# Block means of the values: GpSimd additions over a second load, in place of TensorE passes

## The reference, cut to what matters

```python
k_sum = k.reshape(B, H, nb, block, D).max(axis=3)
v_sum = v.reshape(B, H, nb, block, D).mean(axis=3)     # the block means of the values
scores_l = scale * np.matmul(q, k.transpose(0, 1, 3, 2))
scores_s = scale * np.einsum('bhsd,bhnd->bhsn', q, k_sum) + np.log(block)
...
a = softmax(concatenate([scores_l_masked, scores_s], axis=-1))
v_all = np.concatenate([v, v_sum], axis=2)
return np.matmul(a, v_all)
```

## Time and profile before

| | |
|---|---|
| median of 3 runs | 724.75 us (724.41 to 733.85) |
| the profiled execution: its own time | 723.32 us |
| its span | 721.5 us |
| PE busy | 625.3 us (87%) |
| DVE busy | 354.1 us (49%) |
| ACT busy | 259.9 us (36%) |
| POOL busy | 69.0 us (10%) |

### The profile page before, as it was taken

The page is one execution under the profiler, slowest core; times in us unless marked ns, Lnnn a source line. Parts: engine busy times, 40 slices in busy tenths (PEclk is TensorE's granted clock), DMA queues, the critical chain, the costliest instruction groups (busy, mean ns, idle before and its releaser), DMA issues.

```text
span 721.5 us, 11009 instructions
## 1 busy us (share of the span) xinstructions
PE 625.3 (87%) x3326; PEld 532.1 (74%) x3327; DVE 354.1 (49%) x890; ACT 259.9 (36%) x578; POOL 69.0 (10%) x96
## 2 busy tenths in 40 slices
PE   4899999710879899999849969999999999999994
PEld 3899999610658778878624448898899989988993
DVE  3577775572423452552235286644545454545442
ACT  2676775202313231441101114543344434443330
POOL 3121120015000010100100001002000040000001
PEclk9999999855889999999968988999999999999998
DMA  6444337017831481123150431000100010001001
GB/s 173 94 105 104 83 84 294 1 32 275 301 106 30 145 270 29 32 68 133 44 177 12 173 128 50 1 0 1 45 1 1 0 44 0 0 0 44 0 0 44
DMA packets 58297, 56.38 MB, mean 78 GB/s; under 512 B 43360, under 2 KB 43488, under 8 KB 57504
## 3 DMA queue, kind: packets, MB, share of 16 engines
q1 hardware_dynamic: 52480, 38.93, 17.7%
q0 software_dynamic: 3776, 13.44, 4.8%
q10 hardware_dynamic: 2016, 3.70, 2.3%
HBM read 41.04 MB, written 15.01 MB: 78 GB/s over the span
## 4 chain that ended last, share of the span: by engine, by line
PE 69%; DVE 8%; issue 8%; ACT 5%; DMA 4%; POOL 2%; SPq 2%; DVEq 1%; ACTq 0%; POOLq 0%
PE bank L1451 18%; PE bank L1438 17%; PE bank L1356 9%; PE bank L1328 6%; ACT arena L582 3%; DMA mid<-sorted_x 2%; PE bank L1381 2%; PE bank L1201 2%; DVE parts L935 2%; PE bank L1186 2%; POOL sorted_x L495 1%; PE bank L1210 1%; PE bank L1244 1%; PE bank L1394 1%; PE bank L1316 1%
## 5 line engine op out<-in xcount | busy, mean ns | idle before, releaser
L935 DVE TENSOR_TENSOR parts<-arena,parts 128x512 fp32r<-128x512 f32 (+1 forms) x152 | 111.3, 772 | 99.3 <-ACT parts L709 79.3
L1438 PE MATMUL bank<-parts 128*128 128x384 f32 x768 | 148.2, 342 | 2.1 <-DVE parts L935 2.0
L1451 PE MATMUL bank<-parts 128*128 128x512 f32 x576 | 143.7, 394 | 0.4 <-DVE mid L1095 0.3
L1438 PEld LDWEIGHTS bank<-parts 128*128 128x128 f32 x768 | 137.2, 190 | 8.1 <-DVE parts L935 4.0
L1451 PEld LDWEIGHTS bank<-parts 128*128 128x128 f32 x576 | 106.8, 188 | 21.0 <-DVE mid L1095 1.3
L1356 PE MATMUL bank<-parts 128*128 128x512 f32 x312 | 77.3, 405 | 6.2 <-DVE parts L935 5.3
L1328 PE MATMUL bank<-parts 128*128 128x512 f32 x312 | 76.1, 401 | 2.2 <-DVE parts L935 2.2
L1356 PEld LDWEIGHTS bank<-parts 128*128 128x128 f32 x312 | 59.6, 194 | 20.1 <-issue 4.8
L709 ACT ACTIVATE parts<-arena 128x512 fp32r<-128x512 f32 x64 | 40.4, 631 | 84.1 <-PE bank L1451 84.1
L1328 PEld LDWEIGHTS bank<-parts 128*128 128x128 f32 x312 | 59.0, 193 | 14.6 <-issue 2.8
L935 DVE TENSOR_TENSOR parts<-bank,parts 128x512 fp32r<-128x512 f32 (+1 forms) x56 | 35.2, 649 | 43.0 <-ACT parts L699 20.8
(11 more groups left out here) (171 smaller groups left out, 707.8 us busy)
## 6 DMA issues: line engine op xcount, KB each, us to landing
arena<-in_moe_w SPq DMA_DIRECT2D x24, 512.0 KB, 5.0
sorted_x<-mid POOLq DMA_DIRECT2D x1, 5160.0 KB, 17.5
arena<-in_moe_w_ch SPq DMA_DIRECT2D x2, 2048.0 KB, 8.3
arena<-in_moe_w_ch SPq DMA_DIRECT2D x4, 1024.0 KB, 9.0
mid<-sorted_x ACTq DMA_DIRECT2D x14, 258.0 KB, 3.2
arena<-in_k SPq DMA_DIRECT2D x16, 192.0 KB, 2.7
arena<-in_q SPq DMA_DIRECT2D x16, 192.0 KB, 3.2
x_all<-folded_y SPq DMA_DIRECT2D x6, 512.0 KB, 6.9
```

Source lines behind the costliest of these rows:

```text
L935: return dve.tensor_tensor(out, whole, upper.bitcast(F32), ALU.subtract)
L1438: last = pe.matmul(bank[2 + f % 2][:, 0:GN], w[:, f % 2, r], x[:, par, c, :], start=(c == 0 and w is m1_hi and x is cT_hi), stop=(c == DC ...
L1451: last = pe.matmul(bank[4 + t][:, :], x[:, f % 2, r], w[:, f % 2, :], start=(f == 0 and x is g_hi and w is m2_hi), stop=(f == MC - 1 and w ...
```

## The change

The averaging matrix, the 14 passes, their bank and their semaphore go. A second buffer `blocks` of two halves takes the values of a pair once more, in another layout: one block of 32 positions (32 x 64 numbers, 8 KB) to a partition, 24 partitions for each head, at the very partitions where the means belong in `vB`. GpSimd clears the buffer at the start. For each pair it adds the upper half of a partition's row to the lower half, four times over, and a fifth addition leaves 64 sums in `block_sum`. Each addition waits for the one before. ScalarE copies these sums into `vB` with the factor 1/32. For the first pair VectorE does the sum (a reduction over 32 x 64) and the two copies. The sums of pair i+1 stand on GpSimd right behind its columns of block maxima. The averaging matrix is 896 of the columns of the table of constants, which is now that much shorter.

```diff
@@ SyncE
+            def load_blocks(i, par):
+                for hh in range(2):
+                    lo = WB + (P - HB - NB) * hh
+                    vh = v_dram[bass.ds(2 * i + hh, 1)].rearrange("a (n j) d -> (a n) (j d)", j=BLOCK)
+                    sp.dma_start(blocks[lo:lo + NB, par, :], vh).then_inc(blocks_in[par], 16)
...
             sp.wait_ge(v_cleared, 2)
+            sp.wait_ge(blocks_set, 1)
+            load_blocks(0, 0)
             load_v(0, 0)
+            load_blocks(1, 1)
...
-            def next_pair(i, par):
+            def next_pair(i, par, more=True):
 
                 sp.wait_ge(qk_ps, 3 * (i + 1))
                 load_qk(i + 1)
                 sp.wait_ge(av_ps, ST * i + SIX)
                 load_v(i + 1, 1 - par)
+                if more:
+                    sp.wait_ge(vmean_ok, i + 1)
+                    load_blocks(i + 2, par)
@@ GpSimd
+            pool.memset(blocks, 0.0).then_inc(blocks_set, 1)
             pool.memset(vA, 0.0).then_inc(v_cleared, 1)
...
+            def block_sums(i, par):
+
+                pool.wait_ge(blocks_in[par], 32 * ((i + 2) // 2))
+                pool.wait_ge(vmean_ok, i)
+                pool.sem_inc(waited, 1)
+                n = BLOCK * D // 2
+                for step in range(4):
+                    pool.tensor_tensor(blocks[:, par, 0:n], blocks[:, par, 0:n], blocks[:, par, n:2 * n], ALU.add).then_inc(halved, 1)
+                    pool.wait_ge(halved, 4 * (i - 1) + step + 1)
+                    pool.sem_inc(waited, 1)
+                    n //= 2
+                pool.tensor_tensor(block_sum, blocks[:, par, 0:n], blocks[:, par, n:2 * n], ALU.add).then_inc(vsum_ok, 1)
+
             def keys_and_means(i, par):
                 windows(i, par)
                 block_max_columns(i, par)
+                block_sums(i, par)
@@ ScalarE
             def block_mean_rows(i, par):
 
-                act.wait_ge(vmean_ps, i + 1)
+                act.wait_ge(vsum_ok, i + 1)
                 for hh in range(2):
                     r = slice(WB + WB * hh, WB + WB * hh + WB)
-                    v_mean = Q_BANK[r, D * hh:D * hh + D].rearrange("p (a n) -> p a n", a=1).broadcast_to([WB, ST, D])
-                    last = act.activation(vB[r, par, :, hh, :], v_mean, ACT.Copy)
+                    v_sum = block_sum[r, :].rearrange("p (a n) -> p a n", a=1).broadcast_to([WB, ST, D])
+                    last = act.activation(vB[r, par, :, hh, :], v_sum, ACT.Copy, scale=1.0 / BLOCK)
                 last.then_inc(vmean_ok, 1)
...
-            block_mean_rows(0, 0)
@@ VectorE, ahead of the loop
+            dve.wait_ge(blocks_in[0], 32)
+            dve.tensor_reduce(block_sum, blocks[:, 0].rearrange("p (j d) -> p d j", d=D), axis=AX.X, op=ALU.add).then_inc(vsum_ok, 1)
+            dve.wait_ge(vsum_ok, 1)
+            dve.wait_ge(v_cleared, 2)
+            for hh in range(2):
+                r = slice(WB + WB * hh, WB + WB * hh + WB)
+                v_sum = block_sum[r, :].rearrange("p (a n) -> p a n", a=1).broadcast_to([WB, ST, D])
+                last = dve.tensor_scalar(vB[r, 0, :, hh, :], v_sum, 1.0 / BLOCK, None, ALU.mult)
+            last.then_inc(vmean_ok, 1)
@@ TensorE
-                    pe.wait_ge(v_in[par], 128 * ((i + 2) // 2))
-                    for t in range(ST):
-                        pe.matmul(Q_BANK[:, 0:P], block_mean[:, t, :], vA[:, par, t].rearrange("p h d -> p (h d)"), start=(t == 0), stop=False)
-                    pe.matmul(Q_BANK[:, 0:P], block_mean[:, ST, :], vB[:, par, ST - 1].rearrange("p h d -> p (h d)"),
-                              start=False, stop=True).then_inc(vmean_ps, 1)
...
                 if t == 0:
+                    pe.wait_ge(v_in[par], 128 * ((i + 2) // 2))
                     pe.wait_ge(vmean_ok, i + 1)
...
-                    if t in STAGE_AT and not last_pair:
-                        if t == 0:
-                            pe.wait_ge(vmean_ok, i + 1)
-                        stage(i + 1, 1 - par, STAGE_AT.index(t))
+                    if t < 3 and not last_pair:
+                        stage(i + 1, 1 - par, t)
```

More of the change, by code:

```diff
@@ L51 @@
 T_PRESENT, T_USED, T_COLS = T_EXP + E, T_EXP + E + 1, T_EXP + E + 2
-STAGE_AT = (0, 1, 2, 4)
 GATED = ((), (), (), (), (), (0,)), ((1,), (2,), (3,), (4,), (5, 6), (7, 8))
@@ L80, in shape_constants @@
     cols, at = {}, 0
-    for name, n in (("ident", P), ("mask", 3 * 2 * NS), ("block", 7 * 2 * HB), ("base", NT), ("forced", NT),
+    for name, n in (("ident", P), ("mask", 3 * 2 * NS), ("base", NT), ("forced", NT),
                     ("first", E), ("iota", 1), ("thr", NT), ("tri", E), ("slot", SLOTS + 1), ("ones", 1), ("odd", CW), ("expert", E), ("dest", NT), ("sum", P)):
@@ L100, in shape_constants @@
     put("mask", -np.stack([mask, second], 2))
[L102 to L111, removed]
     token = P * np.arange(NT)[None, :] + np.arange(P)[:, None]
@@ L181, in build @@
         mask = const("mask").rearrange("p (v h s) -> p v h s", v=3, h=2)
-        block_mean = const("block").rearrange("p (t n) -> p t n", t=7)
         class Cut:
@@ L211, in build @@
         xT_gate = mid[:, XW:XW + 1024].rearrange("p (b n) -> p b n", b=2)
+        blocks = mid[:, XW + 1024 + DM:XW + 1024 + DM + 2 * BLOCK * D].rearrange("p (b n) -> p b n", b=2)
         a = Cut(arena)
@@ L274, in build @@
         mean, var, rstd = (s(NT) for _ in range(3))
+        block_sum = s(D)
         fr = Cut(fou)
@@ L294, in build @@
         v_in = pair_of("v_in")
-        qk_ps, qk_sb, kmax_ok, ksum_ok, kwin_ok, vmean_ps, vmean_ok = sems("qk_ps qk_sb kmax_ok ksum_ok kwin_ok vmean_ps vmean_ok")
+        qk_ps, qk_sb, kmax_ok, ksum_ok, kwin_ok, halved, vsum_ok, vmean_ok = sems("qk_ps qk_sb kmax_ok ksum_ok kwin_ok halved vsum_ok vmean_ok")
+        blocks_set, = sems("blocks_set")
+        blocks_in = pair_of("blocks_in")
         s_ps, masked_ok, probs_ok, sum_ok, rinv_ok = sems("s_ps masked_ok probs_ok sum_ok rinv_ok")
@@ L381, in _ @@
                     next_pair(2 * step + par, par)
-            next_pair(PAIRS - 2, 0)
+            next_pair(PAIRS - 2, 0, False)
             w1_d = w1.rearrange("e (c p) n -> e p c n", p=P)
@@ L478, in keys_and_means @@
                 block_max_columns(i, par)
+                block_sums(i, par)
             pool.sem_inc(ksum_ok, 1)
-            keys_and_means(0, 0)
+            windows(0, 0)
+            block_max_columns(0, 0)
             with pool.Fori(0, PAIRS // 2 - 1) as step:
@@ L587, in attend @@
                         stage(i + 1, 1 - par, t - 1)
-                    if t == STAGE_AT[3] + 1 and not last_pair:
+                    if t == ST - 1 and not last_pair:
                         block_mean_rows(i + 1, 1 - par)
@@ L1180, in stage @@
                         last = turn(q_raw, 2 + t, P * t)
-                else:
-                    pe.wait_ge(qk_sb, 3 * i + 3)
-                    pe.wait_ge(consts_in, 16)
-                    pe.wait_ge(v_in[par], 128 * ((i + 2) // 2))
-                    for t in range(ST):
-                        pe.matmul(Q_BANK[:, 0:P], block_mean[:, t, :], vA[:, par, t].rearrange("p h d -> p (h d)"), start=(t == 0), stop=False)
-                    pe.matmul(Q_BANK[:, 0:P], block_mean[:, ST, :], vB[:, par, ST - 1].rearrange("p h d -> p (h d)"),
-                              start=False, stop=True).then_inc(vmean_ps, 1)
-                    return
                 last.then_inc(qk_ps, 1)
@@ L1225, in turn_gate @@
             def turn_gate(n):
-                if n == 0:
-                    pe.wait_ge(vmean_ok, PAIRS)
-                elif n <= EARLY:
+                if 1 <= n <= EARLY:
                     pe.wait_ge(lg_sb, n)
-                else:
+                elif n:
                     pe.wait_ge(xg_sb, n - 1)
@@ L1271, in _ @@
             scores(0, 0, 1)
-            stage(0, 0, 3)
             with pe.Fori(0, PAIRS // 2 - 1) as step:
```

## The result

The changed kernel takes 760.4 us (median of 4 runs, 759.35 to 764.23) against 724.6 us: 1.047 of the kernel before, 95% interval 1.038 to 1.056. The profiled execution has a span of 757.5 us against 721.5. That is slower, as forecast, but by 36 us and not by 21, and above the range.

What follows compares the result with a forecast made beforehand. TensorE was taken to bound the kernel, busy 87% of the span. 723.32 + 16.0 (waits) + 6.8 (clock) - 1.0 (start) = 745.1 us, forecast as 746 us since that execution is 1.43 us below the median; range 733 to 758.

Steps and rivals of the forecast that it cites:

- the order of the links: In each pair: GpSimd's additions behind its block-maxima columns, then ScalarE's rows of means and exponentials, then TensorE's turn; break-even 3.12 us.
- T: GpSimd, start of first addition to end of last: 2.9, 4.5 or 6.6 us by bounds, 5.4 taken.
- The hand-overs: Four waits between GpSimd's five additions, taken at half of 0.17 us each, 0.3 us for four.
- the wait: TensorE's turn of the next pair's first tile comes 2.28 us later; seven waits cost 16.0 us.
- The clock: TensorE idles 3.8 us before the turn; 1.7 us lost per clock fall, 4 of 7 taken, 6.8 us (0 to 11.9).
- The start: Before the loop, clearing, loads, pair 0's means and pair 1's keys: a gain of 1 us, ends -2 and +3.
- The loads in the loop: Two more DMAs of 192 KB in each pair, costed at nothing; without cover about 1 us in a pair.
- rival 1: The same wait before TensorE's turn without any fall of the clock: 739.8 us; chance 0.20.
- rival 2: Cheaper additions on GpSimd, 4.5 us, with one clock fall or none: 734 to 735 us; chance 0.16.
- rival 4: GpSimd's additions end before ScalarE wants them, TensorE's time is saved: 713 us, or 722; chance 0.07.
- rival 3: Dear additions on GpSimd, 6.6 us, and a clock fall in every pair: 760 us; chance 0.09.

Runs made afterwards that it cites:

- the first experiment: The changed kernel with only the fifth addition over 64 elements kept, four halving additions left out; output differs, 15 slots of 128 rows instead of 13; 743.9 us.
- the fourth experiment: The changed kernel with 32 unread turns of the identity on TensorE behind the last values of pairs 0 to 5; 749.2 us, 1.031 of the kernel before.
- the seventh experiment: The kernel before with only GpSimd's clearing of the block buffer and the extra loads, which nobody reads; 729.6 us, 1.006 of the kernel before.
- the second experiment: The changed kernel without the addition over 1024 elements, other four kept; output differs, 15 slots of 128 rows instead of 13; 768.3 us.

## Why the prediction was right or wrong

**Direction and mechanism: right.** The change takes 1.5 us from TensorE in each pair (11.47 against 13.0 us, the first experiment) and puts GpSimd's additions in a chain that costs more. The releaser, the order of the links and their places are as predicted; moving the sums a pair earlier turns the loss into a gain of 1.2 to 1.5%.

**T, the length of the additions: 5.85 us where 5.4 was taken,** inside 4.5 to 6.6. The additions alone were sized rightly, 5.12 us where 5.1 was left for them, at (2.36 - 1.27) us for 512 elements, 2.1 ns each, with 0.18 us fixed. The Trainium skill's price for one addition of 2048 elements (GPSIMD Engine Reference, section 3.1), 4497 ns, agrees: an estimate at the measured rate is 4.5 us. But the prediction's 4.4 us, scaled from it to 1984 elements, leaves out four of the five fixed costs. The hand-overs were mis-sized: 0.18 us each, 0.73 in all, where I took half of a hand-over between engines, 0.3 us in all. Within one engine GpSimd pays as much as between two. T is 0.45 us longer for it, the first addition starts 0.09 later (0.34 us behind the start of L477, 0.25 taken), ScalarE starts 0.14 sooner (0.03 us behind the last addition, 0.17 taken), and its rows and exponentials up to the turn take 0.07 more. So the wait is 2.75 and not 2.28 us; with 3.15 in the second pair of the loop and 2.2 in the last it is 19.2 and not 16.0 us over seven pairs: 3.2 us.

**The clock: the largest error.** I took four falls of seven at 1.7 us, 6.8 us. It fell in every pair; the fourth experiment prices it at 1.85 us in each of six, and 4.8 us lie behind the seventh wait: about 16 us. The step that failed is "whether each gap brings the clock down I cannot read from one case", after which I took about half. It was not one case. The trace of the kernel before has four gaps of more than 2.7 us that TensorE entered at the full clock: that of the earlier trace rows, that before 375.18 shown above, and these:

```profile
203.62 0.69 PE L1316 MATMUL bank<-cst,mid 128*128 128x128 f32 x2 [5.59 <-DMA mid<-sorted_x]
...
428.97 1.33 PE L1428 MATMUL bank<-cst,mid 128*128 128x128 f32 x5 [3.95 <-DVE mid L1108]
```

The clock was down at the end of each of the four or right behind it. So a fall in all seven was what that trace said, and it would have given 11.9 us, 5.1 more. The other 4.3 us are the length of the falls: 1.7 us from the earlier trace rows is near the mean of the six (1.85), but they cost from 1.3 to 2.9 us each, and the seventh 4.8. That a fall could last ten microseconds was to be read too: behind the gap before 428.97 the clock read 0.50 until 439, with two short gaps in it. That the 4.8 us of the last pair are all the clock's was read from its windows, here and in the fourth experiment, and not tried by taking the fall away. Why the clock fell behind two of the gaps of 1.6 us and not behind the others, and why falls are of such different length, stays open.

**The start: the wrong sign.** "I take a gain of 1 us" was a loss of 3.3. The issue of pair 1's keys slipped to 18.99 (the third request for values still took 3.44 us where it took 4.35, and 3.53 in the seventh experiment, which has the long table of constants; so the shorter table is not seen to shorten the queue) and they landed 3.8 us later, not 2.7, behind 4 more loads. VectorE's reduction, which reads with a stride of 64 elements, took 3.62 us and not 2.5, but it ended at 18.45, before the keys were asked for, and is not in that wait. From a gain of 1 to a loss of 3.3 it is 4.3 us.

3.2 + 9.4 + 4.3, less the 2.7 that came back, are 14.2 us: the difference between the 36.0 us by which the span grew and the 21.8 of the forecast. All three errors have one sign, and the range was made as if they were independent. Its upper end does not follow from its words either: T = 6.6 with the middle of the clock's cost gives 724.75 + 24.4 + 6.8 - 1.0 = 755, not 758. The loads in the loop, costed at nothing, cost nothing (the seventh experiment). Rivals 1, 2 and 4 did not happen; the time of rival 3 (760 us) was right by luck: it had every pair's fall of the clock right, its T of 6.6 us was too long, and its start had the wrong sign.

## What to carry to other kernels

An engine that is busy for a sixth of the time is free only at the right moment: ask when its input is there and when its output is wanted, and start the work a whole turn of the loop earlier if its input allows. Price a gap of TensorE of a few microseconds as the gap plus a stretch at half clock behind it, each time, unless the trace shows gaps of that length without a fall; look for all such gaps in the trace, and for how long each fall lasted. A chain of dependent small additions on GpSimd cost its elements plus about 0.36 us a link here, 0.18 fixed and 0.18 of hand-over.

## What the runs showed of the hardware

- The clock fell behind 2 of 6 gaps of 1.5 to 1.6 us (the second experiment), behind all seven gaps of 3.6 to 4.5 us of the changed kernel and all four of 2.8 to 10.8 us that the kernel before entered at the full clock, and held behind gaps of 0.6 to 1.0 us (the fourth). In the last pair it fell 1.2 us after the work had begun again and stayed low for some ten microseconds of dense work, until about 158; in the fourth experiment for over 12. Equal gaps with equal work ahead had different outcomes.
- An addition of two fp32 tensors on GpSimd is 2.36, 1.27, 0.72, 0.45 and 0.32 us for 1024, 512, 256, 128 and 64 elements of 128 partitions, less for 512 elements than the subtraction of a scalar for each partition (1.57 us).
- An instruction of VectorE over 4 elements took up to 1.95 us in place of 0.16 while GpSimd added, and ended when the addition did.
- Sums over 32 elements with a stride of 256 bytes take VectorE 3.62 us for 2048 elements, 1.8 ns each; the maxima over neighbours take 0.95 us for 768, 1.2 ns each.
